# Layer one's input weights and activations moved by 192 bytes, counted modulo 1024

## The reference, cut to what matters

```
attn = softmax(scale * q @ k.T, keys kept: sink or within the window) @ v
x    = attn as (1536, 512)
h    = x @ w_in;  g = max(0.01 * h, h);        x = g @ w_out      # layer one
h    = x @ w_in2; g = h / (1 + exp(-h));       out = g @ w_out2   # layer two
```

## Time and profile before

| | us |
|---|---|
| median of three runs | 608.14 (605.96 to 608.2) |
| the profiled execution's own time | 605.87 |
| its span, first to last instruction | 604.1 |
| TensorE busy | 598.4 (99%) |
| weight loads busy (beside the matmuls) | 507.7 (84%) |
| VectorE, ScalarE, GpSimd busy | 365.4, 305.2, 142.7 |
| granted TensorE clock | 1.0 in all slices |

### The profile page before, as it was taken

The page is one execution under the profiler, slowest core; times in us unless marked ns, Lnnn a source line. Parts: engine busy times, 40 slices in busy tenths (PEclk is TensorE's granted clock), DMA queues, the critical chain, the costliest instruction groups (busy, mean ns, idle before and its releaser), DMA issues.

```text
span 604.1 us, 10156 instructions
## 1 busy us (share of the span) xinstructions
PE 598.4 (99%) x3562; PEld 507.7 (84%) x3562; DVE 365.4 (60%) x808; ACT 305.2 (51%) x666; POOL 142.7 (24%) x194
## 2 busy tenths in 40 slices
PE   9999999999999999999999999999999999999997
PEld 5778888888788888788888889899898989899996
DVE  5865654545556767323685576867677675756562
ACT  6775555564436444323543564646464554635442
POOL 6844443443435152150575000000000000000000
PEclk9999999999999999999999999999999999999999
DMA  8814452634123222130887534443535444445301
GB/s 283 226 61 125 139 156 74 186 100 137 37 53 106 88 78 97 36 113 2 270 288 241 204 110 134 144 143 124 166 121 174 162 149 137 147 142 193 121 0 71
DMA packets 26961, 80.58 MB, mean 133 GB/s; under 512 B 3360, under 2 KB 4512, under 8 KB 26912
## 3 DMA queue, kind: packets, MB, share of 16 engines
q1 hardware_dynamic: 26912, 79.94, 41.4%
HBM read 71.54 MB, written 8.39 MB: 132 GB/s over the span
## 4 chain that ended last, share of the span: by engine, by line
PE 98%; DVE 1%; issue 0%; ACT 0%; DVEq 0%; ACTq 0%
PE y_ps L1338 22%; PE y_ps L1395 22%; PE h_ps L1317 18%; PE s_ps L1346 8%; PE h_ps L1346 8%; PE s_ps L1317 4%; PE o_ps L1279 3%; PE t_ps L1346 3%; PE s_ps L1221 2%; PE t_ps L1246 2%; PE y_ps L1207 1%; PE s_ps L1207 1%; PE o_ps L1292 1%; PE y_ps L1183 1%; PE y_ps L1246 1%; PE y_ps L1279 0%
## 5 line engine op out<-in xcount | busy, mean ns | idle before, releaser
L1338 PE MATMUL y_ps<-g,wout 128*128 128x512 f32 x576 | 146.7, 396 | 0.0
L1395 PE MATMUL y_ps<-wout,g 128*128 128x512 f32 x576 | 139.6, 391 | 0.0
L1395 PEld LDWEIGHTS y_ps<-wout,g 128*128 128x128 f32 x576 | 104.8, 188 | 20.4 <-issue 0.4
L1338 PEld LDWEIGHTS y_ps<-g,wout 128*128 128x128 f32 x576 | 104.0, 188 | 19.7 <-issue 0.7
L1317 PE MATMUL h_ps<-x,win 128*128 128x512 f32 x480 | 118.5, 394 | 0.0
L1317 PEld LDWEIGHTS h_ps<-x,win 128*128 128x128 f32 x480 | 87.3, 188 | 17.4
L978 DVE TENSOR_TENSOR wout<-w_raw,wout 128x512 fp32r<-128x512 f32 x82 | 58.5, 714 | 45.8 <-ACT wout L719 45.8
L680 ACT ACTIVATE prob<-sm,neg_max 128x260 f32<-128x260 f32 (+2 forms) x96 | 42.8, 446 | 77.4 <-DVE sm L887 54.1
L782 ACT ACTIVATE g_f<-c_sum 128x512 f32<-128x512 f32 x24 | 15.2, 633 | 84.8 <-DVE c_sum L1036 84.8
L881 DVE CUSTOM_DVE_ANT_0 sm<-s_ps,mask 128x260 f32<-128x260 f32 (+1 forms) x67 | 27.3, 408 | 49.1 <-PE s_ps L1221 43.8
L983 DVE TENSOR_TENSOR g<-g_f,g 128x512 fp32r<-128x512 f32 x48 | 36.4, 758 | 32.8 <-ACT g L727 32.7
(11 more groups left out here) (151 smaller groups left out, 956.5 us busy)
## 6 DMA issues: line engine op xcount, KB each, us to landing
w_sums<-w_sums SPq DMA_DIRECT2D x32, 640.0 KB, 3.9
w_raw<-w SPq DMA_DIRECT2D x36, 512.0 KB, 3.6
w_raw<-w SPq DMA_DIRECT2D x48, 384.0 KB, 3.0
qk_raw<-qk SPq DMA_DIRECT2D x28, 260.0 KB, 4.6
stage<-w SPq DMA_DIRECT2D x8, 512.0 KB, 5.7
v<-vt SPq DMA_DIRECT2D x12, 256.0 KB, 5.3
y<-qk_raw SPq DMA_DIRECT2D x12, 256.0 KB, 3.2
qk_plain<-qk_first SPq DMA_DIRECT2D x4, 520.0 KB, 4.5
```

What stands on the lines that cost most here:

```text
L1338: ins = mm(y_ps[d][:, :], wout[:, split_slot[split_of[F]], wp, d * P:(d + 1) * P], g[:, gp, F % 2, :], start=(first and wp == HI and gp == ...
L1395: ins = mm(y_ps[d][:, :], g2[:, q % 2, gp, at, d % 2 * P:(d % 2 + 1) * P], wout[:, slot, wp, :], start=(first and wp == HI and gp == HI), ...
```

## The change

A tensor of 192 bytes that nothing uses is put between `x` and `win`, and one of 832 bytes behind `g`. So `win`, `g` and the attention's first inputs `qk_plain` (which reuse the second half of `win` and the front of `g`) begin at 192 modulo 1024 and no longer at 0. All that lies behind `g` moves by 1024 bytes and keeps its place modulo 1024. `xs_odd` is put at `one_at - 192`, and so stays where it was. No instruction is added, removed or moved.

```
         x = sb("x", [P, 2, C, TILES * P], F32R)
+
+
+        sb("skip", [P, 192 // 4], F32)
         one_at = nc.sbuf_base
         win = sb("win", [P, KEPT, 2, HD], F32R)
         g = sb("g", [P, 2, 2, BLK], F32R)
         one_end = nc.sbuf_base
+        sb("fill_up", [P, 832 // 4], F32)
...
-        (xs_odd,), end = over(one_at, ("xs_odd", [7, 2, BLK], F32R))
+        (xs_odd,), end = over(one_at - 192, ("xs_odd", [7, 2, BLK], F32R))
```

## The result

The changed kernel is slower: 609.26 us median of 20 runs (608.49 to 612.65) against 606.3 us for the kernel before on the same chips (20 runs, 605.54 to 608.38); ratio 1.0055, 95% interval 1.0045 to 1.0066, that is +3.3 us. The two medians lie 3.0 us apart: executions fall on two levels some 2.2 us apart (before, 605.5 to 606.5 and 608.0 to 608.4), and the two profiles on the upper one, those of win_only and w7_odd_128, are already 1.9 and 2.0 us behind the profile of before when 10 us have passed. The us that stand beside a ratio are worked out from the ratio. The profiled execution's span is 607.6 us, 3.5 more than before.

What follows compares the result with a forecast made beforehand. TensorE was taken as the bound, with next to no waits. Layer one's loss of 2.3 us, all else 0, on 607.0 us for the kernel before gave 609.3 us; range for 8 in 10: 602.6 to 612.2.

Steps and rivals of the forecast that it cites:

- The bound: Whole kernel: TensorE busy 598.4 of 604.1 us, its four waits 2.3 us, so matmul count times start distance sets the time.
- The choice: Layer one's long matmuls: 192 bytes of distance costs them 4.1 ns each, rather than gaining the short ones' 2.5 ns.
- settled pace: Layer one alone: groups of twelve long matmuls start every 2.72 us, 226.7 ns each, 13.3 over the columns.
- the gain: Rival, layer one: the short matmuls' gain holds for long ones, -4.3 us, 605.0 us; chance 0.34.
- one rhythm: Long matmuls' 226.7 ns and short ones' 120.0 are one fixed rhythm at equal places, 13.3 ns over the columns.
- a wandering: Layer one outside the settled pace: groups of twelve start unevenly, 2.75 to 2.79 us apart.
- The price of 4.1 ns: Each long matmul out of the settled pace: 230.8 - 226.7 ns, from groups that follow short matmuls.
- The term of the sum: Layer one: 624 settled matmuls x 11/12 x 4.1 ns = 2.3 us more; the 528 others 0.
- a dearer rhythm: Rival, layer one: the new distance has its own fixed rhythm, 2.80 us for twelve, +3.8 us, 611.4 us; chance 0.10.
- The level: Runs fall on two levels; the middle, 607.0 us, was taken for the kernel before, giving 609.3 us.
- my own bound of 0.5%: Whole kernel: about 0.5%, 3.0 us, can be told from no change; faster 0.27, slower 0.25, same 0.48.
- What was costed at nothing: Layer two 0, qk_plain at most 0.4 us taken as 0, other engines' work on win and g under 1 us, covered by slack.

Runs made afterwards that it cites:

- win_only: Kernel before with only win moved 192 bytes further on, g unmoved: 606.56 us against 605.95, ratio 1.0004.
- w7_odd_128: Kernel before with only w7_odd moved, by 128 bytes: 606.27 us, ratio 0.9993.
- g_only: Kernel before with only g moved 192 bytes further on, win and qk_plain unmoved: 609.45 us, ratio 1.0044.
- w7_odd_192: Kernel before with only w7_odd moved, by 192 bytes: 605.89 us, ratio 0.9997.
- all_192: Kernel before with every tensor moved 192 bytes further on, all distances kept: 605.9 us, ratio 0.9997.
- after_256: Changed kernel with 256 bytes in place of 192: 606.27 us against 606.57 for the kernel before, ratio 0.9996.
- slots_64: Kernel before with each of the six slots of win and wout 64 bytes further on than the slot before: 610.28 us, one run.
- short_64: Kernel before with layer two's short-matmul inputs at 192 and their weights 64 bytes further on modulo 256: 604.74 us against 606.57, ratio 0.9977.

## Why the prediction was right, and where it was not

**The bound.** TensorE with next to no waits, so that a change of places shows in the distance between starts alone: held. Span +3.5 us, busy +3.5, waits the same.

**The choice.** The trace had two readings that spoke against each other: short matmuls gain 2.5 ns from 192 bytes, and long ones lose when they are out of their settled pace. I took the second for the long ones, and it held; the chance of 0.34 on the gain was the price of having no row with a distance in 512 columns. That both paces are one rhythm was argued; what the runs show is that both lines settle at distance 0 and 256, and run faster at none that was tried. Nor is what lies outside this pace a wandering, as I had it, with groups unevenly 2.75 to 2.79 us apart: at the change's distances both lines repeat a pace of their own. In win_only the matmuls of `hidden` start 229, 232 and 226 ns apart, over and over, and in g_only those of `project` 233 or 234. The price of 4.1 ns came from groups at distance 0 that were catching up after short ones, which is another thing; that it lies between the two lines' prices is luck.

**The term of the sum.** 624 settled matmuls x 11/12 x 4.1 ns = 2.3 us was too small: layer one lost 3.1. The count holds up: 595 matmuls of layer one start 225 to 227.5 ns ahead of the next in the trace before, against the 624 taken, and they lost 2.7 of the 3.1 us. The price was one for both lines and isn't. `hidden` loses (2.74 to 2.76 less 2.72)/12 = 2 to 3 ns, `project` (2.80 - 2.72)/12 = 6.7. For `project` it was the rival that came true, a dearer rhythm of its own at 2.80, which I had given 0.10 on the ground that no two groups in a row kept it before; g_only shows it alone. So the loss of the settled pace is the forecast's, the dearer rhythm in its place is the rival's, at two prices, and the sum fell between: +3.3 us measured, +2.3 forecast, +3.8 for the rival.

**The level.** 609.3 was forecast and 609.26 measured, and that they agree so closely is luck: the kernel before has 606.3 in 20 runs, not the 607.0 that I took, and the medians lie 3.0 us apart, not 2.3; the two errors cancel. By my own bound of 0.5%, 3.0 us, the loss lies on the edge (1.0045 to 1.0066 lies about it), between "same" at 0.48 and slower at 0.25. The gain rival's time has a slip: 4.3 us less than the middle, 607.0, is 602.7 and not 605.0, which is 4.3 less than the forecast; the forecast doesn't hang on it, and the lower end of the range, 602.6, still takes it in.

**What was costed at nothing.** Layer two: 251.5 us before and after. `qk_plain`: what is different ahead of 48 us is 0.4 us and lies in the first 10; w7_odd_192, where `qk_plain` stays, is 0.5 us late there as well; not tried by itself. The work of the other engines on `win` and `g`: no wait of TensorE came of it in the changed kernel's profile.

**The page.** By the Trainium skill, "SBUF — State Buffer", section "Who interferes with whom", TensorE never waits on anyone and has a read port for each operand. The measurement decides against it being the whole story: all_192 and after_256 at 2.72 us and the changed kernel at 2.74 to 2.80 differ in addresses alone.

**Open.** Why 0 and 256 settle, why there are two paces at 192, what decides whether a long group behind short ones comes in settled, and what in the chip has a period of 256 bytes. No run took the load of weights away from beside the stream, so that it is a collision of the two reads is argued, not shown.

## What to carry to other kernels

When TensorE is the bound and nothing else waits, read the start-to-start distance of groups, not durations or busy shares: 0.02 to 0.08 us in a group of twelve was nearly the whole of +0.55%. Check what a padding does for each pair of loaded and streamed operands (modulo 256 for the long matmuls here), and test it in the same shape: what helped 256 columns by 2.5 ns cost 512 columns 2 to 7. A padding that repairs one pair can spoil another that shares a tensor, as `w7_odd` did with its two inputs.

## What the runs showed of the hardware that I had not expected

- Float32r matmuls of 512 columns that follow one another settle at 226.7 ns when loaded and streamed bytes lie 0 or 256 apart (in after_256 both lines do). At 16 and at 240 bytes those that come in settled stay at it and the others don't reach it; at 32, 48, 64, 80, 96, 128 and 144 they take 232 to 234 ns, at 192 229 to 233.
- A group that enters unsettled at distance 0 needs up to nine of its twelve matmuls to settle: 2.73 to 2.77 us for twelve, against 2.72.
- At 192 bytes the same line and shape holds 2.80 us in one run (slots_64) and 2.75 in another (win_only), with the operands in the same places modulo 1024.
- The pace of a long group hangs on the addresses of the short matmuls ahead of it: 2.77 us in the kernel before and 2.72 in short_64, with its own operands unmoved.
